# Two-layer gated network behind an mLSTM: layer two's up products on half rows of TensorE

## The reference

```
rms = sqrt(mean(x * x) + 1e-6);  xn = x / rms * rms_g
g   = xn @ w_gate                 # 1536x320 @ 320x1536
val = xn @ w_val                  # the same size
out = (g * sigmoid(g) * val) @ w_out    # 1536x1536 @ 1536x320
```

## Time and profile before

| | |
|---|---|
| median of 3 runs | 491.52 us (489.08 to 491.59) |
| the profiled execution | 491.35 us, span 489.6 us |
| busy: PE, weight loads | 480.6 us (98%), 467.1 us (95%) |
| busy: DVE, ACT, POOL | 237.4 us (48%), 195.9 us (40%), 110.6 us (23%) |
| layer two on PE | from 289.36 us to the end |

### The profile page before, as it was taken

The page is one execution under the profiler, slowest core; times in us unless marked ns, Lnnn a source line. Parts: engine busy times, 40 slices in busy tenths (PEclk is TensorE's granted clock), DMA queues, the critical chain, the costliest instruction groups (busy, mean ns, idle before and its releaser), DMA issues.

```text
span 489.6 us, 8618 instructions
## 1 busy us (share of the span) xinstructions
PE 480.6 (98%) x3443; PEld 467.1 (95%) x3443; DVE 237.4 (48%) x515; ACT 195.9 (40%) x406; POOL 110.6 (23%) x147
## 2 busy tenths in 40 slices
PE   8889999999999999999999999999999999999997
PEld 3889999999999999999999999999999999999997
DVE  8646984463666265535434527540554055405540
ACT  5377827431552636154416744321332123212320
POOL 7857931111011110100014996000000000000000
PEclk9599999999999999999999999999999999999999
DMA  7662530111021011100241430000000100010001
GB/s 260 222 218 85 160 106 28 57 44 45 29 69 58 18 44 56 45 1 11 88 146 48 152 109 2 0 8 33 1 0 4 40 0 1 0 42 2 0 1 40
DMA packets 11470, 27.83 MB, mean 57 GB/s; under 512 B 1526, under 2 KB 5830, under 8 KB 11430
## 3 DMA queue, kind: packets, MB, share of 16 engines
q1 hardware_dynamic: 11110, 27.20, 17.0%
q10 hardware_dynamic: 320, 0.08, 0.1%
HBM read 25.23 MB, written 1.97 MB: 56 GB/s over the span
## 4 chain that ended last, share of the span: by engine, by line
PE 94%; DVE 3%; ACT 2%; issue 0%; DVEq 0%; ACTq 0%
PE bank L940 21%; PE bank L941 20%; PE bank L943 13%; PE bank L961 9%; PE bank L963 9%; PE bank L962 9%; PE bank L885 5%; PE bank L858 2%; PE bank L813 2%; PE bank L895 2%; PE bank L877 1%; PE bank L833 1%; PE bank L835 1%; ACT L561 1%; DVE d_rhs L741 0%
## 5 line engine op out<-in xcount | busy, mean ns | idle before, releaser
L940 PE MATMUL bank<-x_hi,wgv_hi 128*128 128x256 f32 (+1 forms) x720 | 217.7, 308 | 1.3 <-DVE x_lo L722 1.3
L941 PE MATMUL bank<-x_lo,wgv_hi 128*128 128x256 f32 (+1 forms) x720 | 214.2, 303 | 0.0
L943 PE MATMUL bank<-x_hi,wgv_lo 128*128 128x256 f32 (+1 forms) x480 | 145.6, 303 | 0.0
L940 PEld LDWEIGHTS bank<-x_hi,wgv_hi 128*128 128x128 f32 x720 | 136.6, 190 | 3.1 <-DVE x_lo L722 1.5
L941 PEld LDWEIGHTS bank<-x_lo,wgv_hi 128*128 128x128 f32 x720 | 136.7, 190 | 0.4
L561 ACT ACTIVATE sg<-bank 128x256 f32<-128x256 f32 (+1 forms) x120 | 51.0, 426 | 161.1 <-PE bank L941 160.8
L943 PEld LDWEIGHTS bank<-x_hi,wgv_lo 128*128 128x128 f32 x480 | 91.0, 190 | 0.0
L769 DVE TENSOR_TENSOR hf<-sg,bank 128x256 f32<-128x256 f32 (+1 forms) x120 | 56.8, 473 | 69.8 <-ACT sg L561 67.0
L961 PE MATMUL bank<-wo_hi,h_hi 128*128 128x320 f32 x288 | 89.7, 311 | 0.0
L963 PE MATMUL bank<-wo_hi,h_lo 128*128 128x320 f32 x288 | 89.0, 309 | 0.0
L962 PE MATMUL bank<-wo_lo,h_hi 128*128 128x320 f32 x288 | 89.0, 309 | 0.0
(11 more groups left out here) (108 smaller groups left out, 435.2 us busy)
## 6 DMA issues: line engine op xcount, KB each, us to landing
step<-in_w_gv SPq DMA_DIRECT2D x7, 576.0 KB, 3.8
step<-in_vok SPq DMA_DIRECT2D x12, 324.0 KB, 2.9
step<-in_qk_t SPq DMA_DIRECT2D x24, 160.0 KB
raw_x<-in_w_gv SPq DMA_DIRECT2D x5, 576.0 KB, 5.4
raw_p<-in_w_gv SPq DMA_DIRECT2D x4, 576.0 KB, 5.0
y<-y_tok SPq DMA_DIRECT2D x12, 160.0 KB, 1.8
step<-in_vok SPq DMA_DIRECT2D x10, 180.0 KB, 3.9
step<-in_q_t SPq DMA_DIRECT2D x10, 180.0 KB, 2.4
```

The costliest lines, as they stand in the source:

```text
L940: pe.matmul(ps, wgv_hi[:, wc, s, cs], x_hi[:, xs, s, :], start=(s == 0), stop=False)
L941: mm = pe.matmul(ps, wgv_hi[:, wc, s, cs], x_lo[:, xs, s, :], start=False, stop=(s == 2))
L943: pe.matmul(ps, wgv_lo[:, wc, s, cs], x_hi[:, xs, s, :], start=False, stop=False)
```

## The change

In layer two all up products use 64 rows. The array's lower half (partitions 0 to 63) and upper half (64 to 127) each get a product of their own, issued one after the other: 64 rows, 128 x 384 out, the two in different banks. Two hidden tiles are worked as a pair in four phases. In the "own" phase of a tile the lower half sums its rows of gate, the upper half its rows of value, over all three steps (9 products each; the last step's 64 rows of gate stand in the lower half alone, those of value in the upper half alone). In its "cross" phase the lower half adds its rows of value and the upper half its rows of gate, over two steps (6 each). The order is own f, own f+1, cross f, cross f+1, so that no bank is written from both halves at once; a cross phase waits for `own_done`. A pair takes four banks, and pairs take banks 0 to 3 and 4 to 7 by turns; the down part takes its turn too. The last-step slot of weights is packed anew on the host: chunk 2c has the high parts (gate below, value above), chunk 2c+1 the same, of which POOL makes the low parts. The two transposes move behind the up part of block 0, ahead of its first and second pass of the down part.

The core of the diff:

```diff
+        def half_of(k, turn):
+            return 4 * (((PAIRS + 1) * k + turn + 1) % 2)
+
+        def pair_bank(n):
+            k, f = divmod(n - F1, NF)
+            return half_of(k, f // 2) + 2 * (f % 2)
...
+                else:
+
+                    pool.wait_ge(whi1, c + 1)
+                    pool.tensor_tensor(wgv_lo[:, c, 0, :], r[:, 0, :], wgv_hi[:, c, 0, :].bitcast(F32), ALU.subtract)
+                    last = pool.tensor_tensor(wgv_lo[:, c, 1, :], r[:, 1, :], wgv_hi[:, c, 1, :].bitcast(F32), ALU.subtract)
+                    if c % 2:
+                        last = pool.tensor_tensor(wgv_hi[:, c, 2, :], r[:, 2, :], wgv_hi[:, c, 2, :].bitcast(F32),
+                                                  ALU.subtract)
+                    last.then_inc(split1, 1)
...
+            def hidden_pair(k, i):
...
+                xs = slice(T1 * k, T1 * k + T1)
+                for phase in range(4):
+                    f = 2 * i + phase % 2
+                    n = F1 + NF * k + f
+                    c = f // FC
+                    cs = slice(f % FC * P, (f % FC + 1) * P)
+                    own = phase < 2
+                    if own:
+
+                        if i > 1:
+                            pe.wait_ge(hf_done, n - 3)
+                        elif i == 0:
+                            pe.wait_ge(x2_done, max(T1 * (k + 1), NT - B))
+                            if k == 0:
+                                pe.wait_ge(x_done, NT)
+                            else:
+                                pe.wait_ge(hf_done, n - 1)
+                        elif k == 0:
+                            pe.wait_ge(hf_done, F1)
+                            pe.wait_ge(yo_done, NT)
+                        else:
+                            pe.wait_ge(x2_done, NT)
+                            pe.wait_ge(oe_done, T1 * k)
+                        if k == 0:
+                            pe.wait_ge(split1, 2 * (c + 1))
+                    else:
+                        pe.wait_ge(own_done, 2 * (n - F1 + 1))
+                    steps = [(s, p) for s in range(3 if own else 2) for p in range(3)]
+                    for s, p in steps:
+                        for r in range(2):
+                            m = r if own else 1 - r
+                            ps, done = ((g_view, g_done), (v_view, v_done))[m]
+                            rs = slice(HALF * r, HALF * r + HALF)
+                            if p < 2:
+                                w = wgv_hi[rs, 2 * c + (m if s < 2 else 0), s, cs]
+                            else:
+                                w = wgv_lo[rs, 2 * c + m, s, cs] if s < 2 else wgv_hi[rs, 2 * c + 1, s, cs]
+                            x = (x_hi, x_lo, x_hi)[p][rs, xs, s, :]
+                            last = (s, p) == steps[-1]
+                            mm = pe.matmul(ps(1, n), w, x, start=own and (s, p) == (0, 0), stop=last and not own)
+                            if last:
+                                mm.then_inc(own_done if own else done, 1)
...
-                for f in range(NF):
-                    hidden(1, k, f)
-                    if k == 0 and f in (1, 3):
-                        piece(("O", NT - B + f // 2))
+                for i in range(PAIRS):
+                    hidden_pair(k, i)
                 for t in range(T1):
+                    if k == 0 and t < B:
+
+                        piece(("O", NT - B + t))
                     for half in range(2):
                         project(1, k, t, half)
```

More of the change, by code:

```diff
@@ L38 @@
 F1 = NB0 * NF
+PAIRS = NF // 2
+HALF = P // 2
 PARTS = [(0, 1), (1, 2), (2, 4), (4, NJ)]
@@ L191, in turn_of @@
             return (NF + B) * (n // NF) + n % NF
+        def half_of(k, turn):
[3 more added lines that the diff above has]
+            return half_of(k, f // 2) + 2 * (f % 2)
         def g_view(lay, n):
-            return bank[turn_of(n) % 4][:, 0:N0] if lay == 0 else bank[2 * ((n - F1) % 2)][:, 0:N1]
+            return bank[turn_of(n) % 4][:, 0:N0] if lay == 0 else bank[pair_bank(n)][:, 0:N1]
         def v_view(lay, n):
-            return bank[turn_of(n) % 4][:, N0:2 * N0] if lay == 0 else bank[2 * ((n - F1) % 2) + 1][:, 0:N1]
+            return bank[turn_of(n) % 4][:, N0:2 * N0] if lay == 0 else bank[pair_bank(n) + 1][:, 0:N1]
         def o_view(lay, m):
-            return bank[((NF + B) * (m // B) + NF + m % B) % 4 if lay == 0 else 4 + m][:, 0:DM]
+            if lay == 0:
+                return bank[((NF + B) * (m // B) + NF + m % B) % 4][:, 0:DM]
+            return bank[half_of(m // T1, PAIRS) + m % T1][:, 0:DM]
         def part_of(j):
@@ L249, in mlstm_moe_kernel @@
         x2_done = sem("x2_done")
+        own_done = sem("own_done")
         g_done = sem("g_done")
@@ L265, in mlstm_moe_kernel @@
         whi1 = sem("whi1")
-        wlo1 = sem("wlo1")
         split1 = sem("split1")
@@ L385, in split_gv @@
             def split_gv(lay, c):
-                whi, wlo, split = ((whi0, wlo0, split0), (whi1, wlo1, split1))[lay]
                 r = raw_of(lay, c)
[L388 to L395, removed]
+                if lay == 0:
+                    pool.wait_ge(whi0, c + 1)
+                    for s in range(2):
+                        pool.tensor_tensor(wgv_lo[:, c, s, :], r[:, s, :], wgv_hi[:, c, s, :].bitcast(F32),
+                                           ALU.subtract).then_inc(wlo0, 1)
+                    pool.wait_ge(wlo0, 2 * c + 2)
+                    pool.tensor_tensor(wgv_hi[HALF:P, c, 2, :], r[HALF:P, 2, :], wgv_hi[HALF:P, c, 2, :].bitcast(F32),
+                                       ALU.subtract).then_inc(split0, 1)
+                    pool.wait_ge(split0, c + 1)
+                else:
[6 more added lines that the diff above has]
+                    last.then_inc(split1, 1)
             def split_o(lay, c):
@@ L600, in _ @@
                         h_high(1, F1 + NF * k + f - 1, f - 1)
-                    if k == 0 and f in (1, 3):
-                        piece(("O", NT - B + f // 2))
                 h_high(1, F1 + NF * k + NF - 1, NF - 1)
                 for t in range(T1):
+                    if k == 0 and t < B:
+                        piece(("O", NT - B + t))
                     act.wait_ge(o_done, NT + T1 * k + t + 1)
+                    if k == 0 and t:
+                        act.wait_ge(ot_done, NT - B + t)
                     if k:
                         act.wait_ge(out_sent[t], 16 * k)
-                    act.activation(y_tok[:, t, 0:DM], o_view(1, t), ACT.Copy).then_inc(oe_done, 1)
+                    act.activation(y_tok[:, t, 0:DM], o_view(1, T1 * k + t), ACT.Copy).then_inc(oe_done, 1)
         @block.vector
@@ L802, in _ @@
                         h_low(1, n - 1, f - 1)
-                    if k == 0 and f in (1, 3):
-                        piece(("O", NT - B + f // 2))
                 h_low(1, F1 + NF * k + NF - 1, NF - 1)
+                if k == 0:
+                    for t in range(B):
+                        piece(("O", NT - B + t))
         @block.tensor
@@ L907, in piece, with hidden @@
                         pe.wait_ge(r_exp, 2 if n == 0 else 3)
+                    if n == NT - B:
+                        pe.wait_ge(hf_done, F1 + NF - 2)
                     turn(bank[7], 1 + n % B).then_inc(ot_done, 1)
-            def hidden(lay, k, f):
+            def hidden(k, f):
                 c, i = f // FC, f % FC
[L912 to L931, removed]
+                n = NF * k + f
+                if f == 0:
+                    pe.wait_ge(x_done, B * k + B)
+                if turn_of(n) >= 4:
+                    k0, f0 = divmod(turn_of(n) - 4, NF + B)
+                    if f0 < NF:
+                        pe.wait_ge(hf_done, NF * k0 + f0 + 1)
+                    else:
+                        pe.wait_ge(yo_done, B * k0 + f0 - NF + 1)
+                xs = slice(B * k, B * k + B)
                 if k == 0 and i == 0:
-                    pe.wait_ge((split0, split1)[lay], 2 * (c + 1))
+                    pe.wait_ge(split0, 2 * (c + 1))
                 cs = slice(i * P, (i + 1) * P)
@@ L936, in hidden @@
                     ps, done = ((g_view, g_done), (v_view, v_done))[m]
-                    ps = ps(lay, n)
+                    ps = ps(0, n)
                     wc = 2 * c + m
@@ L951, in project @@
                         pe.wait_ge(hf_done, n0 + NF - 4 + t + 1)
-                    elif k:
-                        pe.wait_ge(oe_done, T1 * (k - 1) + t + 1)
+                    else:
+                        pe.wait_ge(hf_done, n0 + NF - 2)
                 ts = slice(t * P, (t + 1) * P)
-                ps = o_view(lay, B * k + t if lay == 0 else t)
+                ps = o_view(lay, (T1 if lay else B) * k + t)
                 for f in range(half * NF // 2, (half + 1) * NF // 2):
@@ L977, in _ @@
                     if slot < NF:
-                        hidden(0, k, slot)
+                        hidden(k, slot)
                     else:
@@ L1028, with up_chunks @@
```

(11 more changed lines are left out.)

## The result

| | before | after |
|---|---|---|
| median of 4 runs | 491.47 us (489.08 to 491.59) | 483.88 us (482.21 to 484.59) |
| the profiled execution | 491.35 us, span 489.6 us | 484.59 us, span 482.8 us |
| layer two on PE, first to last product | 197.2 us | 190.2 us |

The ratio is 0.985, with a 95% interval from 0.981 to 0.989: faster by 1.5%. The forecast was 486.6, with 480 to 492 around it.

A forecast was written before the change was run, and what follows sets the result against it. PE, busy without a gap in layer two, was taken as the bound, so product count and step matter. From 491.35 us, -6.5 + 1.5 - 0.04, about -4.9, gave 486.4; plus 0.17 for the median, 486.6 us, range 480 to 492.

The forecast's parts named there:

- The step of a pair: Layer two's up part: two half products take 0.176 us, 720 such steps replacing 768 of 0.1734; 6.5 us saved.
- the S piece: Earlier mLSTM products alternating between half rows: 0.112 us a pair, 3 ns over a full product, taken over for layer two.
- The crossings: Going into or out of half rows, in and out once per layer-two block: 0.19 us each, 1.5 us added.
- The waits for `own_done`: Cross phases on PE: 9 or 6 pairs stand between, 1.58 or 1.06 us against 0.33 needed; nothing added.
- the end of the up part: Layer two's results come bunched; last `h_low` at T + 3.5, asked for at T + 4.8, cover 1.3 us; nothing added.
- transposes and POOL: Moved transposes exposed as before, 0.04 us wait gone; about 4 us of POOL work saved, worth nothing to the total.
- rival 2: Layer two: one half's top hides behind the other's columns; pair 0.170 to 0.160 us, 474.9 us at best; chance 0.09.
- the top counted per half: Layer two: the 13 ns over the columns count for each half; pair up to 0.187 us, 494.1 us; chance 0.14.
- the 0.1774: Layer two's pair in us, by the skill's about 4 ns per further row tile; sum 1.0 us above the forecast's.
- the 0.226: Layer two's pair in us, at the skill's yield of 3.07 for four row tiles; 522 us in all.
- Loads in turn: Layer two: the halves' weight loads go one after the other; pair 0.218 us, 516.7 us in all; chance 0.05.
- Columns in turn: Layer two: the halves' columns stream one after the other; pair 0.347 us, 609 us in all; chance 0.04.

The follow-up runs named there:

- runs with 256 and 128 columns: Against the changed kernel, layer two's up products stream only 256 or 128 of their 384 columns; 447.21 and 438.49 us, one run each.
- run with 32 steps: Changed kernel with one more pair of products in each own phase; median 490.38 us against 491.38 of the kernel before, ratio 1.000.
- nine in a row: Changed kernel with, in each phase, all lower-half products issued first, then all upper-half ones (RUN = 9); 508.2 us, one run.
- three in a row: Changed kernel with three lower-half products issued, then three upper-half ones, and so on (RUN = 3); 481.94 us, one run.

## Why the prediction was right

*The step of a pair.* Forecast 0.176 us, measured 0.1733. The mechanism was right and this term mis-sized, by 720 x 0.0027 = 1.9 us: I carried over 3 ns from the S piece, where the loads bound the pair. The runs with 256 and 128 columns show that it goes once the columns bind. With 0.1733 the sum is 720 x 0.1733 = 124.8 instead of 133.2, -8.4.

*The crossings.* Forecast 0.19 each, 1.5 us, from a single S piece; measured 0.20 each, 1.6, at the eight of layer two and again amid the up part.

*What was costed at nothing.* The waits for `own_done`, the end of the up part (last `h_low` at T + 3.75 for my T + 3.5, asked for at T + 5.0 for my T + 4.8, cover 1.3 us as forecast), transposes and POOL added nothing. The run with 32 steps gives only their balance: 198.56 us where 197.2 + 1.6 would be 198.8, so 0.2 us less, of which the forecast had 0.04. That "everything behind is in order" holds at a wait, where all of PE stood for 0.39 us, but not for the products of the two halves (nine in a row).

*The sum.* The recorded terms, -6.5 + 1.5 - 0.04, add up to -5.04 and not to the -4.9 that was carried on, a slip of 0.1 us. With the measured terms the sum is 491.35 - 8.4 + 1.6 = 484.6 us, and the profiled execution took 484.59. That they agree to 0.1 us is in part chance: layer two was 0.2 us shorter than the terms say, and it began 0.2 us later than before (289.53, 289.36). The median of the four runs, 483.88, lies 0.7 below, within their spread (482.21 to 484.59).

*The number.* The range of 480 to 492 reached from rival 2 to no change at all, so that the total fell into it says little for the mechanism. The step from pair to pair and the run with 32 steps say it.

*The rivals.* A step of 0.187 (the top counted per half) or of 0.160 (the top hidden) is excluded at 384 columns, and at 256 by 0.120. So are the 0.1774 and the 0.226 that the prediction gave beside its own terms: the products of a pair start side by side, and the step is that of one. Loads in turn would have made 0.218; they go side by side down to 128 columns. Columns in turn would have made 0.347. My reserve that the earlier trace rows couldn't exclude this last one was right: with 128 columns the pair is load-bound and says nothing of the columns.

## What to carry to other kernels

A last step that fills only half of the array's rows with distinct work can be saved by giving each half products of its own, in different banks; a pair then costs one full product, and 8 steps become 7.5. It pays by steps saved against crossings: here 48 x 0.173 us against 8 x 0.20. In layer one, where a pair of tiles would save 2 x 0.120 = 0.24 us and full-row pieces are woven between nearly all steps, one visit out and back costs 0.40; that is an estimate, not run. Where one half must wait for the other, put another phase between: a wait for the products just issued cost 0.39 us, and with six or more pairs between none was listed.

## What the runs showed of the hardware

Products of different halves are not kept in program order: one half ran about three products ahead of the other (nine in a row: 24.3 of 60 side by side; three in a row: all). So the end of a product of one half doesn't tell that an earlier one of the other half has ended, or even begun (411.11 and 411.64 above); each half needs a semaphore update of its own, as this kernel has for own and cross. And two half-row weight loads side by side take no longer than one: 0.112 us a pair at 128 columns, beside 0.109 for one full load with few columns.
